# Masked linear attention with gated MLPs on one core: the causal mask as a select on GpSimd instead of a product on TensorE

## What is computed

```python
# attention, for every token t, per head
m_new = maximum(f_gate[t] + m, i_gate[t])
f_stab = exp(f_gate[t] + m - m_new); i_stab = exp(i_gate[t] - m_new); m = m_new
C = f_stab * C + i_stab * outer(v[t], k[t])
n = f_stab * n + i_stab * k[t]
y[t] = sigmoid(o_gate[t]) * (C @ q[t]) / maximum(abs(n @ q[t]), 1)
# first MLP
xn = x / sqrt(mean(x*x) + 1e-6) * rms_g
x = (silu(xn @ w_gate) * (xn @ w_val)) @ w_out
# second MLP
h = x @ w_in
x = (maximum(h, 0) + alpha * minimum(h, 0)) @ w_out2
```

## Time and profile before

| | us |
|---|---|
| timed runs, median of 3 | 523.59 (521.03 to 525.62) |
| profiled execution, its own time | 525.28 |
| its span, first to last instruction | 523.5 |
| PE busy in the span | 494.2 |
| DVE, ACT, POOL busy | 359.5, 204.0, 233.3 |

### The profile page before, as it was taken

One profiled execution on the slowest core, in us unless ns is written; L12 is line 12 of the kernel. 1 busy time (PEld: TensorE's weight loads), 2 busy tenths in 40 slices (PEclk: granted clock), 3 DMA queues, 4 the chain that ended last, 5 costly groups with the idle time before them and its releaser, 6 DMA issues.

```text
span 523.5 us, 9899 instructions
## 1 busy us (share of the span) xinstructions
PE 494.2 (94%) x3113; PEld 468.1 (89%) x3113; DVE 359.5 (69%) x710; ACT 204.0 (39%) x508; POOL 233.3 (45%) x250
## 2 busy tenths in 40 slices
PE   5988889999999999999999999999999999998996
PEld 3877888998999999998998989998998999988995
DVE  7475598749989656438989656447989732248784
ACT  1331434444544323234553423233553422234452
POOL 3340357742755424331764524332664622225664
PEclk9565799999999999999999999999999999999999
DMA  7744642032442390002342392002333320004462
GB/s 121 174 86 56 154 152 92 3 86 55 111 109 84 101 159 19 1 1 57 97 119 68 91 164 45 0 0 52 78 111 90 86 64 2 0 4 101 120 139 95
DMA packets 80725, 41.14 MB, mean 79 GB/s; under 512 B 51548, under 2 KB 80684, under 8 KB 80684
## 3 DMA queue, kind: packets, MB, share of 16 engines
q1 hardware_dynamic: 80684, 40.65, 35.2%
HBM read 38.67 MB, written 1.97 MB: 78 GB/s over the span
## 4 chain that ended last, share of the span: by engine, by line
PE 40%; issue 25%; DVE 14%; POOL 11%; DMA 4%; ACT 2%; SPq 0%; POOLq 0%; DVEq 0%; ACTq 0%
PE bank L956 20%; PE bank L964 8%; POOL hidT L834 5%; POOL w L826 4%; PE bank L967 4%; PE bank L922 3%; DMA shared<-in_moe_w_in 2%; DVE win L709 2%; DVE u L739 2%; DMA shared<-in_moe_w_out 1%; POOL decay_rhs L801 1%; DVE hid L742 1%; PE bank L910 1%; PE bank L917 1%; PE bank L928 1%
## 5 line engine op out<-in xcount | busy, mean ns | idle before, releaser
L834 POOL TENSOR_TENSOR hidT<-hid,hidT 128x384 fp32r<-128x384 f32 x112 | 118.3, 1056 | 233.0 <-ACT hidT L494 232.1
L494 ACT CAST hidT<-hid 128x384 fp32r<-128x384 f32 x112 | 57.5, 513 | 142.8 <-DVE hid L722 91.8
L956 PE MATMUL bank<-x2T,win 128*128 128x384 f32 x512 | 100.5, 340 | 2.4 <-DVE win L709 1.6
L956 PEld LDWEIGHTS bank<-x2T,win 128*128 128x128 f32 x512 | 87.3, 188 | 4.7 <-DVE win L709 2.0
L716 DVE SCALAR_TENSOR_TENSOR u<-th,bank 128x384 f32<-128x384 f32 x48 | 26.6, 554 | 87.7 <-ACT th L516 84.8
L956 PE MATMUL bank<-xT,wg 128*128 128x384 f32 x384 | 76.6, 342 | 3.6 <-DVE u L716 2.8
L956 PE MATMUL bank<-xT,wv 128*128 128x384 f32 x384 | 76.0, 340 | 0.0
L964 PE MATMUL bank<-w,hidT 128*128 128x320 f32 x384 | 69.6, 316 | 5.1 <-POOL w L826 4.7
L956 PEld LDWEIGHTS bank<-xT,wg 128*128 128x128 f32 x384 | 66.8, 191 | 5.2 <-issue 3.1
L964 PEld LDWEIGHTS bank<-w,hidT 128*128 128x128 f32 x384 | 58.4, 188 | 12.1 <-POOL w L826 11.1
L956 PEld LDWEIGHTS bank<-xT,wv 128*128 128x128 f32 x384 | 67.0, 189 | 1.1 <-DVE hid L722 0.3
(11 more groups left out here) (127 smaller groups left out, 679.3 us busy)
## 6 DMA issues: line engine op xcount, KB each, us to landing
shared<-in_moe_w_out SPq DMA_DIRECT2D x38, 320.0 KB, 5.4
shared<-in_moe_w_in SPq DMA_DIRECT2D x34, 256.0 KB
shared<-in_moe_w_in SPq DMA_DIRECT2D x34, 128.0 KB
q_in<-in_q SPq DMA_DIRECT2D x12, 160.0 KB, 4.4
k_in<-in_k SPq DMA_DIRECT2D x12, 160.0 KB, 4.7
v_in<-in_v SPq DMA_DIRECT2D x12, 160.0 KB, 4.7
o_in<-in_o_gate SPq DMA_DIRECT2D x12, 160.0 KB, 4.3
shared<-in_moe_w_gate SPq DMA_DIRECT2D x6, 256.0 KB
```

The source lines that it names most:

```text
L494: a.copy(hidT[:, i % NH, 0], hid[:, i % 2]).then_inc(s_hid_hi, 1)
L834: gp.tensor_tensor(hidT[:, i % NH, 1], hid[:, i % 2], hidT[:, i % NH, 0].bitcast(F32), ALU.subtract).then_inc(s_hid_lo, 1)
L956: last = te.matmul(dst, w[:, blk, col:col + P], x[:, part, xb, :], start=(n == 0), stop=(n == len(terms) - 1))
```

## The change

The mask product of line 901 goes, with maskF and maskR and what fills them. The exponential is taken of the decay exponents alone, and GpSimd then sets dx to 0 where the key is behind the query, with an affine select of 128x512 for each half of the heads, in steps D1 and S. DVE's pT waits for the select instead of the exponential. GpSimd's two decay products of the next block move from D1 and S to state and inter. The warm-up products read identR twice.

```diff
-            elif what in ("D1", "S") and g < G - 1:
-                decay(n + 1, g + 1, int(what == "S"))
+            def causal(n, half):
+                pool.wait_ge(s_dx, 2 * n + half + 1)
+                pool.sem_inc(s_causal_due, 1)
+                gp.affine_select(out=dx[:, half], in_=dx[:, half], compare_op=ALU.is_ge, fill=0.0, base=0,
+                                 pattern=[[0, H // 2], [1, CH]], channel_multiplier=-1).then_inc(s_causal, 1)
...
+                elif what in ("D1", "S"):
+                    causal(n, int(what == "S"))
+                elif what in ("state", "inter") and g < G - 1:
+                    decay(n + 1, g + 1, int(what == "inter"))
...
-                        dve.wait_ge(s_dx, 2 * n + half + 1)
+                        dve.wait_ge(s_causal, 2 * n + half + 1)
...
-                    te.matmul(quad(A[2 * half]), decay_lhs[0:KQ, g * CH:(g + 1) * CH], decay_rhs[0:KQ, half::2, :], start=True, stop=False)
-                    te.matmul(quad(A[2 * half]), identR[:, :], mid(maskR[:, :], P, H // 2, CH), start=False, stop=True).then_inc(s_D_mm, 1)
+                    te.matmul(quad(A[2 * half]), decay_lhs[0:KQ, g * CH:(g + 1) * CH], decay_rhs[0:KQ, half::2, :], start=True, stop=True).then_inc(s_D_mm, 1)
...
-            vec.tensor_copy(maskR[:, :], maskF[:, :]).then_inc(s_const_dve, 1)
```

More of the change, by code:

```diff
@@ L191, in program @@
         identR = sb("identR", [P, P], F32R)
-        maskF = sb("maskF", [P, P])
-        maskR = sb("maskR", [P, P], F32R)
         sel = sb("sel", [P, H])
@@ L246, in program @@
         s_dx = sem("s_dx")
+        s_causal_due = sem("s_causal_due")
+        s_causal = sem("s_causal")
         s_S_mm = sem("s_S_mm")
@@ L296, in program @@
         s_group = [sem(f"s_group{g}") for g in range(G)]
-        N_CONST, N_CONST_DVE, GATE_STEPS = 14, 15, 3 * G + 6
+        N_CONST, N_CONST_DVE, GATE_STEPS = 12, 14, 3 * G + 6
         BACK = 3
@@ L781, in _ @@
                 pool.sem_inc(held, BACK)
-            for ap, value in ((ident[:, :], 0.0), (maskF[:, :], 0.0), (sel[:, :], 0.0), (minus_half[:, :], -0.5),
+            for ap, value in ((ident[:, :], 0.0), (sel[:, :], 0.0), (minus_half[:, :], -0.5),
                               (q_in[:, :, :, D:HP], 0.0), (k_in[:, :, :, D:HP], 0.0), (kw[:, :, D:HP], 0.0), (v_in[:, :, :, D:DA], 1.0)):
                 gp.memset(ap, value).then_inc(s_const, 1)
-            pool.wait_ge(s_const, 8)
+            pool.wait_ge(s_const, 7)
             gp.affine_select(out=ident[:, :], in_=ident[:, :], compare_op=ALU.not_equal, fill=1.0, base=0,
                              pattern=[[-1, P]], channel_multiplier=1).then_inc(s_const, 1)
-            gp.affine_select(out=maskF[:, :], in_=maskF[:, :], compare_op=ALU.is_ge, fill=-BIG, base=0,
-                             pattern=[[1, P]], channel_multiplier=-1).then_inc(s_const, 1)
             for r in range(4):
-                pool.wait_ge(s_const, 10 + r)
+                pool.wait_ge(s_const, 8 + r)
                 gp.affine_select(out=sel[:, :], in_=sel[:, :], compare_op=ALU.not_equal, fill=1.0, base=-32 * r,
@@ L864, in _ @@
             for _ in range(WARM_UP):
-                te.matmul(quad(GV[1]), identR[:, :], mid(maskR[:, :], P, 4, CH), start=True, stop=True)
+                te.matmul(quad(GV[1]), identR[:, :], mid(identR[:, :], P, 4, CH), start=True, stop=True)
             def att(what, g, t):
```

## The result

The changed kernel took 532.67 us in the median of 4 runs (531.04 to 536.17), the kernel before 522.31 beside it (520.33 to 525.62). The ratio is 1.020, with a 95% interval of 1.012 to 1.028: 10 us slower. The forecast was 524.0 with a range up to 529.5, so it is wrong, and by much more than its working allowed.

What follows compares the result with a forecast made beforehand. PE was taken as the bound, nearly full after a low-clock start. From the profiled 525.28: -2.35 masks, +3.75 pile-up, -1.0 start gives 525.7, 0.4 slower, so 524.0 at the median; range 521 to 527, with rivals 518.8 to 529.5.

Steps and rivals of the forecast that it cites:

- the pile-up: Second block of each tile: select and two decays in a row on GpSimd delay DVE's subtractions and pT; 3.75 us lost.
- Part 4: Start, tile 0's three blocks alone: shorter waits gain 1.35 us, less 0.35 for PE's clock; 1.0 us gained.
- Part 3: Second block of each overlapped tile: pT late behind select and two decays, PE loses 1.25 us, 3.75 in all (2.4 to 5.1).
- Part 1: Overlapped tiles: 10 of 18 removed mask products count at 0.235 us each, 2.35 us gained; third block's count 0.
- Part 2: GpSimd selects of 128x512: 0.62 us each, 15 us for 24, hidden in first and third blocks.
- nothing after gives it back: Second block: PE's 1.25 us loss at inter stays, since pT, update and x2 copies follow in the same order.
- I take 0.35 for that (0 to 1.5): Start: us lost if fewer PE columns cost the short full-clock stretch or shift the rise at the first gate.
- The subtractions did wait for GpSimd: Against the rival that the port is no obstacle and all 18 masks count: 518.3 us, chance 0.15.
- the passes did gain 2.2 us: Against the rival that masks were hidden nearly everywhere, so removal gains 0 in the overlapped tiles: 526.3 us, chance 0.12.
- the select took 0.64 us: Against two rivals: select dear at 1.1 us (525.9, chance 0.12) or slow per element at 5 us (some 584, chance 0.03).
- the counts are as planned: Against the rival that the change does not do what it says; it is in the last 0.02.
- an unlucky clock at the start or a place that I missed: Chance of 0.05 within the 0.12 for a result slower by over 1% (5.2 us).

Runs made afterwards that it cites:

- experiment 3: Kernel before without the mask product of line 901 and nothing in its place, causal mask inside a block left out: 523.02 us, ratio 1.003.
- experiment 1: Changed kernel with GpSimd's two decay products waiting until DVE has written both halves of pT: 523.76 us, ratio 1.0027.
- experiment 6: Kernel before, mask product and decay products kept in place, with the selects added and pT waiting for them: 523.78 us, ratio 1.0063.
- experiment 2: Changed kernel with six useless 512-column PE products before inter's wait in the second block of the passes: 526.18 us, ratio 1.0098.
- experiment 5: Changed kernel with decay products held until pT is written, plus one useless 512-column product behind each D0 and D1 of tile 0: 519.97 us, ratio 0.998.
- experiment 4: Kernel before, mask product kept, no select, only the decay products moved from D1 and S to state and inter: 528.22 us, ratio 1.0129.
- experiment 10: Changed kernel, decay pile-up kept, with one useless 512-column product behind each D0 and D1 of tile 0: 528.53 us, ratio 1.0181.
- experiment 9: Changed kernel with decays held for pT, start filler behind tile 0's D0 and D1, and second win chunk's split moved behind x2 transposes: 521.92 us, ratio 1.0016.

## Why the prediction was wrong

The balance, each term from its runs: mask products taken off the passes -2.2 (profiles of experiment 3); select without the pile-up +0.7 (experiments 1 and 3; experiment 6 gives +2.3 with one decay behind it); the pile-up's wait +2.4 (experiments 1 and 2); the clock behind it +6.5 (experiment 2); the clock in the start +3.8 (experiments 1 and 5). Sum +11.2, measured +10.4. The three terms in the middle are steps between the same four medians and add up by themselves; what the sum tests is the rest: -2.2 and +3.8 make 1.6, and experiment 3 measured 1.2.

The step that failed is the price of the clock. Part 4 put it at 0.35 us, where the runs show 3.8, and Part 3 put nothing for it behind the longer wait, where they show 6.5. These two are about all of the 10 us between the forecast (+0.4) and the result (+10.4); the terms of parts 1 to 3 for products, select and wait were off by less than 1 us together.

- Part 1, the products that go: right. 2.2 us against 2.35, pass by pass 0.3, 0.9 and 0.95 against 0.47, 0.94 and 0.94. So the third block's products were worth nothing there, as said. Next to the earlier trace rows the waits simply grew, in the same place of the changed kernel to 0.43 and 0.18 us:

```profile
261.09 1.15 PE L968 MATMUL bank<-w,hidT 128*128 128x320 f32 x6 [0.43 <-POOL w L831]
...
264.49 1.15 PE L968 MATMUL bank<-w,hidT 128*128 128x320 f32 x6 [0.18 <-POOL w L831]
```

- Part 2, the select: right. The group shows a mean of 0.67 and the line a median of 0.64 us against 0.62. In tile 1's first block DVE's second pT waited 1.43 us for a select queued behind a weight split of 1.57 us, as forecast, and PE did not wait for it. The Trainium skill's 12 cycles per element for data-dependent branching ("GPSIMD Engine Reference", section "3.1 Elementwise — side-by-side cycle accounting") don't describe this select: that would be 5.1 us, an estimate.
- Part 3, the pile-up: the mechanism and the idle time right, 1.54 us against 1.7. Its price per pass was 1.07 us of idle time instead of 1.25 (one subtraction took 0.62 us beside the select, not 1). What I had not seen is what idle time does there. "nothing after gives it back" was true; that it would take more was the miss.
- Part 4, the start: xn took 0.90 us as forecast (about 0.9). The first gate product came 0.5 us earlier instead of 1. The mechanism was named rightly, the short stretch at full clock in block two and the later rise at the first gate; both are in the profiles. Its size failed: "I take 0.35 for that (0 to 1.5)". It measures 3.8 us in the start, and 6.5 more came in the passes, where I had no such term at all. The prediction gives no working for the bound of 1.5, and the range rested on it. The range was too narrow by its own terms as well: with masks at 0, pile-up at 5.1 and clock at 1.5 the upper end is 523.6 + 5.1 - 1.35 + 1.5 = 528.8, not 527.

Of the rivals none came true. The subtractions did wait for GpSimd, the passes did gain 2.2 us, the select took 0.64 us, and the counts are as planned (24 products fewer on PE). None of them named the clock; the only chance it had was part of the 0.05 for "an unlucky clock at the start or a place that I missed".

Two things could have been read from what lay there. The profiled execution of before (525.28) was one of its slower runs, and I carried the 1.7 us to the median without asking what they were. By the clocks they were most likely the start's: the profiled one had 0.960, most runs have 0.970, which is some 10 us more at full clock (an estimate: 0.01 of 523.5 us, at a difference of 0.5). So the trace that I worked from had one stretch of about 3.5 us to lose in the start, and the typical run had more. And in the earlier trace rows PE had already 0.47 us of idle time, with nine short transposes of 128 columns behind it; I priced another microsecond there at its own length.

The Trainium skill says that idle gaps between bursts of matmuls bring the clock down ("TensorE: Matmul & The Clock Gate", section "HAM oscillation — how this bites in real kernels"). The traces agree in kind. Here the clock fell behind idle times of 1.2 to 1.5 us ahead of inter, in five of nine passes (experiments 4 and 10, the changed kernel), and in none of the profiles in which that wait was shorter or filled.

What stays open: why the clock falls in one pass and not in the next one with the same gap, in the same execution. Experiments 4 and 10 had it in passes 1 and 2, the changed kernel's profile in pass 3. In the first two the start had been mostly at full clock (0.82 and 0.72 from 12 to 60 us), in the last not (0.51); that this matters is not shown. And whether the pile-up's clock cost is also felt at the last tile's x2 steps (the short dip at 476 us), which hold no edited instruction. PE's waits there are the same in the kernel before (0.39, 0.35 and 0.67 us against 0.40, 0.35 and 0.67), whose clock stayed up; the dip was seen in one profile only and not tried.

## What to carry to other kernels

On an engine whose clock follows its work, price idle time by what follows it as well: taking 4.6 us of idle time out of three places gave 8.9 us here, and six products per pass that compute nothing gave 6.5 us back. Before taking "free" work off such an engine, look at the clock of every run, not of one profile, and find out whether the profile is a typical one. And when operations are moved "later" on a side engine, look at what they then stand next to: the select by itself cost little (0.7 us, and 2.3 with a decay product behind it), the two moved decay products cost most of the 10 us, and one wait undid that.

## What was not expected of the hardware

- Work of no use can pay: 6 products of 512 columns in the start gave 3.8 us (523.76 to 519.97), 6 per pass in front of inter 6.5 us (532.67 to 526.18).
- The low clock came within 2 us behind the gap and held for 6 to 10 us (118 to 124, 241 to 247, 364 to 374, 119 to 129, 242 to 252 in three kernels), though PE was busy all of that time.
- The spread of the kernel before (517.4 to 526.0 us) goes with its mean clock (0.984 to 0.958). That such a spread comes from the start is seen in two other kernels, those of experiments 5 and 9, which are the same up to the first gate product: it came at 54.53 us at a mean clock of 0.57 from 12 to 60 us, and at 52.24 at 0.68.
- Beside a GpSimd operation in progress a DVE subtraction of two SBUF tensors ended just behind it, whether that operation reads one tensor (the select: 0.62 instead of 0.29 us) or two (1.03).
